# A recurrent attention layer and two expert layers on one core: transposes of x and state product moved behind the second-layer products

## The reference

```python
m_new = max(f_gate + m, i_gate)
C = f_stab * C + i_stab * outer(v, k)        # state of a head, 40 x 40
n = f_stab * n + i_stab * k
y = sigmoid(o_gate) * (C @ q) / max(abs(n @ q), 1)
x = y as (3072 tokens, 320)
h = x @ w_in                                  # 320 -> 2048
g = h where h >= 1, 0 where h <= -1, (h + 1)**2 / 4 between
x2 = g @ w_out                                # 2048 -> 320
# then: the best of 8 experts for each token, relu(x2 @ w1[e]) @ w2[e], times its gate
```

## Time and profile before

| | |
|---|---|
| median of 3 runs | 852.54 us (852.46 to 853.27) |
| the profiled execution's own time | 852.34 us |
| its span in the trace | 850.5 us |
| TensorE busy | 768.5 us, 90% |
| VectorE busy | 626.3 us, 74% |
| ScalarE busy | 405.1 us, 48% |
| GpSimd busy | 313.8 us, 37% |
| chain that ended last, TensorE's share | 74% |

### The profile page before, as it was taken

One profiled execution on the slowest core, in us unless ns is written; L12 is line 12 of the kernel. 1 busy time (PEld: TensorE's weight loads), 2 busy tenths in 40 slices (PEclk: granted clock), 3 DMA queues, 4 the chain that ended last, 5 costly groups with the idle time before them and its releaser, 6 DMA issues.

```text
span 850.5 us, 17185 instructions
## 1 busy us (share of the span) xinstructions
PE 768.5 (90%) x5762; PEld 744.7 (88%) x5762; DVE 626.3 (74%) x1010; ACT 405.1 (48%) x651; POOL 313.8 (37%) x296
## 2 busy tenths in 40 slices
PE   2798999999999999999999999805999999999994
PEld 1788999999999999999999999805999999999994
DVE  5575979888898989888888885436676777776750
ACT  3024454444444444444544445405566666766851
POOL 3352534534445453434444434323042333222111
PEclk9999999999999999999999999957899999999998
DMA  7942222223232322232222200057764335527200
GB/s 205 314 138 73 75 88 80 90 84 92 83 97 86 94 76 87 72 87 72 87 72 87 86 1 17 1 165 202 216 205 140 117 99 183 178 90 230 97 20 5
DMA packets 40273, 91.28 MB, mean 107 GB/s; under 512 B 6781, under 2 KB 24321, under 8 KB 38826
## 3 DMA queue, kind: packets, MB, share of 16 engines
q1 hardware_dynamic: 36346, 81.69, 31.2%
q0 software_dynamic: 3888, 9.08, 3.8%
HBM read 105.63 MB, written 9.33 MB: 135 GB/s over the span
## 4 chain that ended last, share of the span: by engine, by line
PE 74%; DVE 14%; DMA 4%; issue 3%; ACT 3%; SPq 1%; DVEq 0%; POOLq 0%; POOL 0%; ACTq 0%
PE bank L1251 17%; PE bank L1263 17%; PE bank L1439 12%; PE bank L1387 6%; PE bank L1206 5%; PE bank L1197 3%; PE bank L1401 3%; DVE w_l L1052 2%; PE bank L1214 2%; PE bank L1223 2%; DVE g_l L936 2%; ACT w_h L717 1%; DVE den L885 1%; DVE num L882 1%; DVE xs L896 1%
## 5 line engine op out<-in xcount | busy, mean ns | idle before, releaser
L509 POOL TENSOR_TENSOR g_t<-u_t,r_t 128x512 f32<-128x512 f32 x96 | 134.7, 1403 | 270.4 <-ACT u_t L644 270.4
L639 ACT ACTIVATE r_t<-bank,neg 128x512 f32<-128x512 f32 x96 | 66.0, 688 | 201.4 <-PE bank L1251 201.4
L1263 PE MATMUL bank<-wo_h,g_h 128*128 128x328 f32 x384 | 127.3, 332 | 1.2 <-DVE g_l L936 1.2
L1263 PE MATMUL bank<-wo_l,g_h 128*128 128x328 f32 x384 | 120.1, 313 | 0.0
L1263 PE MATMUL bank<-wo_h,g_l 128*128 128x328 f32 x384 | 120.1, 313 | 0.0
L930 DVE TENSOR_SCALAR u_t<-bank 128x512 f32<-128x512 f32 x96 | 65.4, 681 | 57.4 <-ACT r_t L639 36.9
L575 POOL DMA_INDIRECT out_x<-ob,idx_tok x31 | 37.4, 1206 | 181.6 <-ACT ob L753 170.0
L644 ACT ACTIVATE u_t<-u_t,half 128x512 f32<-128x512 f32 x96 | 69.5, 724 | 55.2 <-DVE u_t L930 55.2
L860 DVE TENSOR_TENSOR_SCAN W<-W,cst 128x512 f32<-128x512 f32 x48 | 84.2, 1757 | 1.9 <-DMA W<-decays 1.9
L1251 PE MATMUL bank<-xT_h,wi_h 128*128 (+1 forms) x384 | 77.8, 284 | 1.6 <-issue 1.6
L1439 PE MATMUL bank<-w_h,h_h 128*128 128x320 f32 x248 | 78.1, 315 | 1.1 <-DVE h_l L1072 1.1
(11 more groups left out here) (211 smaller groups left out, 1969.3 us busy)
## 6 DMA issues: line engine op xcount, KB each, us to landing
raw<-in_w SPq DMA_DIRECT2D x12, 1280.0 KB
W<-decays SPq DMA_DIRECT2D x24, 512.0 KB, 5.1
raw<-in_w SPq DMA_DIRECT2D x12, 1024.0 KB
raw2n<-in_w SPq DMA_DIRECT2D x7, 1280.0 KB
raw1n<-in_w SPq DMA_DIRECT2D x7, 1024.0 KB
raw<-in_w SPq DMA_DIRECT2D x24, 256.0 KB
qG<-in_q SPq DMA_DIRECT2D x24, 180.0 KB
qT<-in_qt SPq DMA_DIRECT2D x48, 80.0 KB
```

The source lines that it names most:

```text
L509: pool.tensor_tensor(g_t[p % 2][:, :], u_t[p % 2][:, :], r_t[p % 2][:, :], ALU.add).then_inc(sm["g_done"], 1)
L639: act.activation(r_t[p % 2][:, :], bank_h[p % 2][:, :], ACT.Relu, bias=neg1[:, 0:1]).then_inc(sm["r_done"], 1)
L1263: mm = pe.matmul(bank_acc[tt][:, 0:DL], l[p % 4][:, c], r[:, f, :], start=f == 0 and a == 0, stop=f == NT1 - 1 and a == 2)
```

## The change

In parts 3 and 7 of a step `turn_x` and `to_state` of the unit stand behind `second`, not in front of it. The other quarters of the recurrence stay where they are, and so do the instructions of the other engines.

```diff
                     first(t, p)
-                    if att and p % 4 != 1:
+                    if att and p % 4 in (0, 2):
                         attention(t + 1, p // 4, p % 4)
                     if prev and p == 5:
                         rank(t - 1)
@@
                     elif prev:
                         second(t - 1, NP1 - 2 + p)
+                    if att and p % 4 == 3:
+                        attention(t + 1, p // 4, 3)
```

## The result

| | before | changed |
|---|---|---|
| median of 10 runs | 853.38 us | 858.52 us |
| ratio, with its 95% interval | | 1.0048 (1.0033 to 1.0064) |
| the profiled execution: time, span | 852.34, 850.5 us | 858.83, 857.0 us |
| a loop step (median of steps 2 to 10) | 40.81 us | 41.23 us |

The change costs 0.48%, some 4 us of 853, by the ratio, and 5.1 us by the two medians. The forecast was no change; the time lies outside its range and on the side of rival B.

What follows compares the result with a forecast made beforehand. TensorE was taken to bound the loop steps. Steps 2 to 10 gain 0.6 us, step 0 gains 0.2, step 1 loses 1.1: 0.3 lost, so 852.7 us (chance 0.50), range 850.2 to 857.0.

Steps and rivals of the forecast that it cites:

- rival B: First product of each step: three waits, address steps and restart add 0.35 at 11 boundaries, 3.9 us, 856.6; chance 0.24.
- TensorE bounds the steps: Loop steps: TensorE busy 39.95 of 40.84 us, so its stalls are paid in full.
- Unit 0 gains 0.97 us a step: Part 3: the wait for xs goes, 1.0 us of cover left; gain 0.95 to 1.04 a step.
- Unit 1 loses 0.90: Part 7 to next step: x's path exposed, 3.99 us against 3.09; loss 0.77 to 1.05 a step.
- back to TensorE: Step boundary: handover from x_low's end to TensorE's first product, put at 0.06 to 0.15 us.
- first handover: Step boundary: x_high's end to x_low's start, semaphore and address step on VectorE, put at 0.04 to 0.15 us.
- Restart 0.06: Step boundary: TensorE's restart after the stall, 0.06 us added to the 2.12 of x's path.
- Nothing in part 2: Part 2: no term in the sum; the delay of new_state and the VectorE work behind it was costed at nothing.
- rival C: Part 0's scans: Vp at 4.33, scan at 4.29, a toss; second scan caught too, xs late, 8 us, 860.8; chance 0.05.
- Step 0 gains 0.2, step 1 loses 1.1: First two steps: step 0 keeps 1.4 and loses 1.24; step 1 gains nothing at unit 0, loses 1.02 at its end.
- The sum: Whole kernel: steps 2 to 10 gain 0.6, step 0 gains 0.2, step 1 loses 1.1; together 0.3 us lost.
- The range: Whole kernel's time: 850.2 to 857.0 us, leaving out the 860.8 case, the large gain and outer parts of two rivals.

Runs made afterwards that it cites:

- e3_wait_last: Changed kernel with TensorE's wait for xl_ready put last, behind r_done and u_done, at a step's first product: 856.09 us, ratio to before 1.0048.
- e2_unit1: Kernel before with only part 7 (unit 1) having transposes and state product behind the second layer: 869.37 us, ratio 1.0196.
- e5_split: Changed kernel with both units' state product back in front of the second layer, only the transposes behind it: 879.15 us, ratio to before 1.0291.
- e7_both: Changed kernel with the xl_ready wait last and GpSimd's table transfers ahead of part 7's addition: 854.17 us, ratio to before 0.9999.
- e9_after_table: Changed kernel with only GpSimd's two table transfers issued ahead of part 7's addition: ratio to before 1.0031, step 40.98 us.

## Why the prediction was wrong, step by step

- **TensorE bounds the steps:** right, each change of a wait came out in the step.
- **Unit 0 gains 0.97 us a step:** right. Measured 1.01 (part 3 shorter by 1.08, 0.07 paid at the first layer behind), 0.99 alone. xs arrived in time. The late state, loads and x_low cost nothing, as forecast.
- **Unit 1 loses 0.90:** this is the step that failed, and in it the term "back to TensorE". The mechanism was right, eleven waits of L1251 for x_low, only its size was off: 1.20 in part 7 and 0.13 more at the restart, 1.33. Link by link: transposes to x_high 0.62 for 0.68, x_high 0.54, first handover 0.16 for at most 0.15, x_low 0.74 for 0.73, and **the handover back to TensorE 0.40, where the sum had 0.06 to 0.15**. I had taken it from TensorE's wait for xs, behind which the next instruction needs no register. Rival B named this place and this reason and put 0.24 on it; by its own measure (0.35 more per boundary) it was right for the ten boundaries in the loop, where 0.34 more passed than at step 11, and the order of the two was mine to weigh better.
- **Restart 0.06:** 0.13, in the first pair (0.51 us for 0.40).
- **Nothing in part 2:** wrong, by 0.09 against the kernel before (step 3) and by 0.26 against a step without this wait (6.42 for 6.16). The tie that rival C described did not occur: Vp and the scan both came 0.24 later in the step (at 3.97 and 4.54 of it, for 3.73 and 4.29), so the scan still started 0.57 us behind Vp and took 3.13. It did not delay xs beyond its cover, but it held the weighted scores, a reader that I had not followed. The kernel before already paid 0.14 there (6.30 for 6.16).
- **Step 0 gains 0.2, step 1 loses 1.1:** right. Step 0's first product to step 1's: 68.83 to 108.82, 39.99 for 40.26, 0.27 gained; step 1: 40.84 for 39.63, 1.21 lost.
- **The sum:** steps 2 to 10 take 370.9 us for 367.5, so 3.4 more (the last of them only 0.1, as the boundary into step 11 is the short one), with the two first steps 4.4 us by the profiles, for the 4.1 that the ratio gives (0.48% of 853). The forecast had 0.3. The spans of the two profiles are 6.5 us apart; 1.9 of that lies behind the start of step 11, a stretch that varies between 333.3 and 336.5 us over this case's profiles.
- **The range** reached to 857.0, and rival B's own value was 856.6, 3.9 above the forecast, where 4.1 to 5.1 were measured. The kernel before took 853.38 in the ten runs, 0.8 more than the 852.54 that the forecast started from; that is part of the distance to the range, not of the change. What separates forecast and result is ten boundaries with some 0.3 us each of unpriced work behind a wait, the restart, and part 2.

## What to carry to other kernels

When a product moves behind other work, price both ends: what it no longer waits for, and what now waits for it. A handover between engines was shortest here where constants stood behind the wait. In a loop, count what the sequencer still has to do there, and try the wait that comes last at the end of the list; where all is constant that order was the slower one (0.15 us for 0.06). And before covering a wait, ask why the data was late: here an edit on a third engine, with no move on the busy one, took away the same microsecond. Lastly, look at the granted clock before a longer wait is called cheap.

## What the runs showed of the hardware

- The same wait of TensorE was answered 0.06 us after its releaser's end with nothing of the sequencer behind it (step 11), 0.15 with a semaphore wait of its own in front of the weight load (step 11 of `e3_wait_last`), 0.20 with one register step behind it and 0.40 with two register steps and a semaphore wait.
- That work is exposed even while TensorE's products still run (0.40 at 267.22), so covering only the releaser's end is not enough.
- With idle times of 1.63 to 2.01 us at the boundaries the granted clock dropped to its lower level behind 6 of 11, for 3.4 or 6.8 us, 2.8 us lost in the worst; with up to 1.40 us it dropped behind none of the changed kernel's 11.
- In step 0 the clock rose to its upper level between 70.7 and 73.4 us in nine of the twelve profiles, and at 78.2 to 78.7 in the others (`e2_unit1`, `e5_split`, `e7_both`), which by estimate cost these some 2 us of step 0 (41.74 us in `e7_both` for 40.08 in `e9_after_table`, which differ otherwise by one reordered wait).
- A VectorE scan of 1.22 us took 3.13 when GpSimd's product Vp was first, and the copy and the addition that GpSimd had queued behind it also went ahead; GpSimd's addition of 1.3 took 1.84 when the scan was first.
